# A fused attention and two mixtures of experts: the first two tiles of each mixture taken as early snapshots

## The reference

```python
# attention: 4 batches x 8 heads x 576 positions x 64, block-causal mask (blocks of 64)
attn = softmax(mask(q @ k.T / 8)) @ v
x = attn.transpose(0, 2, 1, 3).reshape(2304, 512)      # N tokens x D

# first mixture: 8 experts, F = 1024, capacity 576
logits = x @ w_gate;  e = argmax(logits);  g = softmax(logits)[e]
# tokens in order: the first 576 of each expert are kept, the others give 0
y = g * (relu(x @ w1[e]) @ w2[e])

# second mixture, on y as x
do = (x @ w_skip) > 0                                  # tokens that are computed at all
out = x;  out[do] = x + g * (relu(x @ w1b[e]) @ w2b[e])
```

## Time and profile before

| | us |
|---|---|
| median of three runs | 697.13 (696.61 to 699.2) |
| the profiled execution | 697.51 |
| its span, first to last instruction | 696.0 |
| PE busy | 675.1 (97%) |
| DVE / ACT / POOL busy | 365.4 / 263.2 / 144.0 |
| a tile of mixture 1, of mixture 2 (steady) | 14.6, 13.1 |
| mean granted TensorE clock | 0.996 |

### The profile page before, as it was taken

How to read it: one execution, slowest core, us unless ns; L and a number is a source line. 1 busy time by engine, 2 the same in 40 slices (tenths; PEclk the granted TensorE clock), 3 DMA queues, 4 the chain that set the end, 5 groups by cost and what they waited for, 6 DMA issues and landing times.

```text
span 696.0 us, 16986 instructions
## 1 busy us (share of the span) xinstructions
PE 675.1 (97%) x5624; PEld 593.1 (85%) x5625; DVE 365.4 (52%) x1019; ACT 263.2 (38%) x642; POOL 144.0 (21%) x236
## 2 busy tenths in 40 slices
PE   7999999999999799999999999999899999999997
PEld 6788888888887699999899988998798989999986
DVE  3767787787877533357633367435612444411144
ACT  5566566566663122244322143123211433411133
POOL 5100021021011313222222222231212112112112
PEclk9999999999999999999999999999999999999999
DMA  8757568658331354110711158871481688701101
GB/s 179 197 144 197 173 164 240 178 148 252 69 101 70 105 201 147 31 46 24 259 42 39 45 193 321 292 282 43 129 301 60 200 312 326 279 30 45 45 17 33
DMA packets 94332, 103.75 MB, mean 149 GB/s; under 512 B 63629, under 2 KB 63629, under 8 KB 94288
## 3 DMA queue, kind: packets, MB, share of 16 engines
q1 hardware_dynamic: 83600, 79.19, 36.5%
q0 software_dynamic: 9072, 22.89, 9.9%
q10 hardware_dynamic: 1616, 1.08, 0.5%
HBM read 83.44 MB, written 26.53 MB: 158 GB/s over the span
## 4 chain that ended last, share of the span: by engine, by line
PE 88%; DMA 5%; DVE 3%; issue 2%; SPq 1%; ACT 0%; POOL 0%; POOLq 0%; ACTq 0%; DVEq 0%
PE ps L1408 29%; PE ps L1415 24%; PE ps L1304 8%; PE ps L1255 6%; PE ps L1279 5%; PE ps L1311 3%; PE ps L1235 3%; DMA rows<-queue 3%; PE ps L1247 2%; PE ps L1386 2%; PE ps L1397 2%; PE ps L1391 1%; PE ps L1272 1%; DMA queue<-pad 1%; DMA kn<-in_k 1%
## 5 line engine op out<-in xcount | busy, mean ns | idle before, releaser
L1408 PEld LDWEIGHTS ps<-xT,w 128*128 128x128 f32 x1344 | 153.8, 192 | 6.8 <-issue 3.5
L1408 PE MATMUL ps<-xT,w 128*128 128x128 f32 x1344 | 155.2, 275 | 3.9 <-issue 1.4
L984 DVE SCALAR_TENSOR_TENSOR hT_lo<-ps,hT_hi 128x512 fp32r<-128x512 f32 x64 | 44.1, 691 | 134.3 <-ACT hT_hi L1160 129.5
L1415 PE MATMUL ps<-w_hi,hT_hi 128*128 128x512 f32 x256 | 105.2, 411 | 1.2 <-DVE hT_lo L984 1.0
L1415 PE MATMUL ps<-w_lo,hT_hi 128*128 128x512 f32 x256 | 100.6, 393 | 0.0
L1415 PE MATMUL ps<-w_hi,hT_lo 128*128 128x512 f32 x256 | 100.2, 391 | 0.0
L1160 ACT ACTIVATE hT_hi<-ps 128x512 fp32r<-128x512 f32 x64 | 37.9, 593 | 133.3 <-PE ps L1408 133.3
L1408 PE MATMUL ps<-xT,w_last 128*128 128x128 f32 x704 | 81.8, 275 | 0.0
L1408 PEld LDWEIGHTS ps<-xT,w_last 128*128 128x128 f32 x704 | 81.0, 192 | 0.9
L1101 ACT ACTIVATE probs<-ps,negmax 128x128 f32<-128x128 f32 (+3 forms) x128 | 65.8, 527 | 22.1 <-DVE negmax L737 22.1
L737 DVE TENSOR_REDUCE negmax<-ps 128x2 f32<-128x256 f32 (+1 forms) x64 | 51.1, 821 | 33.6 <-PE ps L1260 33.6
(11 more groups left out here) (174 smaller groups left out, 886.1 us busy)
## 6 DMA issues: line engine op xcount, KB each, us to landing
w2all<-in_moe_w SPq DMA_DIRECT2D x10, 2048.0 KB, 14.6
w<-in_moe_w SPq DMA_DIRECT2D x7, 2048.0 KB, 9.0
rows<-queue POOLq DMA_DIRECT2D x38, 257.0 KB, 3.0
w2all<-in_moe_w SPq DMA_DIRECT2D x16, 512.0 KB, 5.2
w<-in_moe_w SPq DMA_DIRECT2D x12, 512.0 KB, 3.8
w_last<-in_moe_w SPq DMA_DIRECT2D x3, 2048.0 KB, 9.0
qn<-in_q SPq DMA_DIRECT2D x32, 144.0 KB, 3.7
out<-pad SPq DMA_DIRECT2D x4, 1152.0 KB, 8.8
```

The lines of the kernel that those rows point to most:

```text
L984: vec.scalar_tensor_tensor(out=hT_lo[:, hs, :].bitcast(f32r), in0=hTp[half], scalar=0.0, in1=hT_hi[:, hs, :], op0=ALU.max, op1=ALU.subtrac ...
L1408: last = mm(hTp[half][:, j, :], w1s[slot][:, c, f:f + P], xT[:, c, :], start=(c == 0), stop=(c == DC - 1))
L1415: last = mm(yp, h_[:, j, :].bitcast(f32r), w_[:, j, :].bitcast(f32r), start=(j + n == 0), stop=(j == FC - 1 and n == 2))
```

## The change

What it does:
- The first tiles of **two** experts (0 and 1) of each mixture are tiles 0 and 1 whatever they hold. They are loaded as snapshots before the last routing has placed its rows, and both 128-row stretches are then blanked with pads in the queue. Where the stretch was full at the snapshot, the expert goes on behind it; where it was not, it is visited again from its first row, in which only the later rows are left.
- `find_early` is gone; `find_full` (five small DVE instructions, once a mixture) gives the table which of the two was full.
- PE: tile 0's hidden matmuls stand around the last `rows_back` and ranks, in place of filler; tile 1 is written out ahead of the loop, on every engine; in mixture 1 the transposes of y and the logits stand between eighths of the second hidden half, and the ranks behind the first eighth of the values.
- DVE: the index part of the last routing stands between `split_h` 0 and 1 of tile 0 (mixture 1); `make_table` stands behind both in both mixtures. A tile's routing is cut in two, around `split_h` 1.
- ACT: the last routing's exp stands behind `copy_x`; pads of experts 5 to 7 behind tile 0's two `relu`, in a loop. SP: pads of experts 0 to 4, in a loop.
- POOL: mixture 1's last batch is scattered once both stretches are blanked; `placed` counts the scatters into queue 2 apart from those into `out`.

The core of the diff:

```diff
-            def load_first(phase, found, placed, rows):
+            def load_firsts(phase, there):
+
 
                 p = ph[phase]
-                sp.wait_ge(p.early_ready, found)
-                sp.sem_inc(carried, 1)
-                late = sp.value_load(tab(phase, T_PAD, LATE), min_val=0, max_val=1)
-                sp.wait_ge((scattered, ph[0].scattered)[phase], late * rows + placed)
-                sp.sem_inc(carried, 1)
-                sp.wait_ge(p.first_padded, late * 16 + 16)
-                sp.dma_start(firsts[phase], queues[phase][0:P, :]).then_inc(p.tile0_loaded, 16)
+                sp.wait_ge((scattered, placed)[phase], there)
+                for e in range(FIRSTS):
+                    sp.dma_start(firsts[phase][e], queues[phase][e * REGION:e * REGION + P, :]).then_inc(p.first_loaded[e], 16)
+                for e in range(FIRSTS):
+                    sp.wait_ge(p.first_loaded[e], 16)
+                    sp.dma_start(queues[phase][e * REGION:e * REGION + P, :], pad[:, :]).then_inc(p.blanked, 16)
...
                 p = ph[phase]
                 if phase == 1:
-                    total = sp.value_load(tab(0, T_CUM, E), min_val=1, max_val=NT)
-                    load_first(1, total, total * 32 + (ENDPADS - 32), 16)
-                pad_ends(sp, phase, range(E // 2, E), p.padded)
+                    total = sp.value_load(tab(0, T_CUM, E), min_val=FIRSTS, max_val=NT)
+                    load_firsts(1, total * 16)
+
+                sp.wait_ge(p.blanked, 16 * FIRSTS)
+                pad_ends(sp, phase, 0, E - ACT_PADS, p.padded)
                 sp.wait_ge(p.table_ready, 1)
...
+                pool.wait_ge(p.first_loaded[0], 16)
+                take_row(0, firsts[phase][0][:, kept].unsqueeze(1))
+                if phase == 0:
+
+                    pool.wait_ge(p.blanked, 16 * FIRSTS)
+                    scatter_batch(B - 1)
                 pool.wait_ge(p.rows_ready, 1)
-                first_rows = [row_of(t) for t in range(1, RING + 1)]
+                first_rows = [row_of(t) for t in range(FIRSTS, FIRSTS + RING)]
                 if phase:
-
-                    pool.wait_ge(ph[0].scattered, total * 32 + (ENDPADS - 16))
+                    pool.wait_ge(placed, total * 16 + 16)
                     carry()
                 else:
                     pool.wait_ge(scattered, B * (NI * 16))
                 pool.wait_ge(p.scattered, ENDPADS)
-                pool.wait_ge(p.padded, 16 * (E - 1))
-                pool.wait_ge(p.first_padded, 32)
-                load_rows(first_rows[0], slice(1, 2))
-                if phase:
-                    scatter(out, y2[:, 0:D], idxo[:, 0:1], N - 1, ph[0].scattered)
+                pool.wait_ge(p.padded, 16 * E)
+                load_rows(first_rows[0], slice(2, 3))
+                if phase == 0:
+                    pool.wait_ge(out_cleared, 16 * B)
+                pool.wait_ge(p.first_loaded[1], 16)
+                take_row(1, firsts[phase][1][:, kept].unsqueeze(1))
+                total = pool.value_load(tab(phase, T_CUM, E), min_val=FIRSTS, max_val=NT)
+                for t in range(3, FIRSTS + RING):
+                    pool.wait_ge(p.loaded, 16 * (t - FIRSTS))
+                    load_rows(first_rows[t - FIRSTS], slice(t % RING, t % RING + 1))
+                if phase == 0:
+                    scatter_values(1)
                 else:
-                    pool.wait_ge(out_cleared, 16 * B)
-                pool.wait_ge(p.tile0_loaded, 16)
...
-                signal(ph[phase].early_ready, value)(vec.tensor_scalar(tab(phase, T_PAD, LATE), count, float(P) - 0.5, None, ALU.is_lt))
+            def find_full(count):
+
+                link(vec.tensor_tensor(full[:, 0:FIRSTS], count[:, 0:FIRSTS], base[:, 0:FIRSTS], ALU.subtract))
+                link(vec.tensor_scalar(full[:, 0:FIRSTS], full[:, 0:FIRSTS], float(P) - 0.5, None, ALU.is_ge))
+                link(vec.tensor_tensor(onward[:, :], full[:, 1:E + 1], full[:, 0:E], ALU.subtract))
+                link(vec.tensor_scalar(onward[:, :], onward[:, :], float(P), float(REGION), ALU.mult, ALU.add))
+                link(vec.tensor_scalar(begun[:, :], full[:, 0:1], float(P), None, ALU.mult))
...
-                link(vec.tensor_scalar(n_[:, 0:1], n_[:, 0:1], 1.0, None, ALU.max))
-                vec.tensor_scalar(tabs[phase][:, T_N, 0:1], n_[:, 0:1], -1.0, None, ALU.add)
+                link(vec.tensor_tensor(n_[:, 0:E], n_[:, 0:E], full[:, 0:E], ALU.subtract))
+                vec.tensor_copy(tabs[phase][:, T_N, 0:E], n_[:, 0:E])
 
                 link(vec.tensor_copy(tmp[:, E + 1:2 * E + 1], n_[:, 0:E]))
...
-                vec.tensor_copy(tabs[phase][:, T_CUM, 1:E + 1], cum_[:, 1:E + 1])
-                link(vec.tensor_scalar(tmp[:, 0:E], n_[:, 0:E], -float(P), float(REGION), ALU.mult, ALU.add))
+                vec.tensor_scalar(tabs[phase][:, T_CUM, 1:E + 1], cum_[:, 1:E + 1], float(FIRSTS), None, ALU.add)
+                link(vec.scalar_tensor_tensor(out=tmp[:, 0:E], in0=n_[:, 0:E], scalar=-float(P), in1=onward[:, :],
+                                              op0=ALU.mult, op1=ALU.add))
                 link(vec.tensor_tensor(past[:, :, :], tile_no[:, 0, :].unsqueeze(2).to_broadcast([P, 32, E]),
...
+                        route_end(t)
+
+                        dve.wait_ge(p.y_taken, t)
+                    else:
+
+                        dve.wait_ge(p.scattered, t * 16 + ENDPADS)
+                    finish_tile(t)
+                    dve.sem_inc(carried, 1)
+                    split_next(t, *ahead)
+
+
+                if phase == 0:
+                    split_h(0, 1)
+                    dve.wait_ge(ranks_ready, B)
+                    last_router.take_rows()
+                    last_router.keep_capacity()
+                    dve.wait_ge(x_scaled, 2 * PAIRS)
+                    index_batch(B - 1)
+                    last_router.count_rows()
+                    make_ends(0)
+                    split_h(1, 2)
+                else:
+                    split_h(0, 1)
+                    split_w2(slice(0, 1), 0, range(2, 4))
+                    split_h(1, 2)
+                make_table(phase)
+                total = dve.value_load(tab(phase, T_CUM, E), min_val=FIRSTS, max_val=NT)
                 if phase:
-                    split_w2(0, 0, range(2, 4))
-                split_h(1, 2)
-                total = dve.value_load(tab(phase, T_CUM, E), min_val=1, max_val=NT)
-                if phase:
-                    dve.wait_ge(ph[0].scattered, done * 32 + ENDPADS)
-                else:
-                    find_early(1, count2[0:1, 0:1], 1)
-                ahead = look_ahead(0)
+                    dve.wait_ge(ph[0].scattered, done * 16 + ENDPADS)
+                    dve.wait_ge(placed, done * 16 + 16)
                 finish_tile(0)
-                split_next(0, *ahead)
+                split_w2(slice(1, 2), 4)
+                tile(1)
...
-                    split_w2(0, 0, range(2), ph[1])
-                    route_tile(total, last=True)
+                    find_full(count2)
+
+                    split_w2(slice(0, 1), 0, range(1), ph[1])
+                    route_begin(total)
+                    split_w2(slice(0, 1), 0, range(1, 2), ph[1])
+                    route_end(total)
+                    make_ends(1)
...
+                if phase == 0:
+                    copy_x(1)
+                    act.sem_inc(p.xq_copied, 1)
+                    router_exp(NI, shifted_ready, exps_ready, B)
+                relu(0, 0)
+                relu(0, 1)
+                pad_ends(act, phase, E - ACT_PADS, E, p.padded)
+                copy_x(2)
                 act.sem_inc(p.xq_copied, 1)
-
-                pad_ends(act, phase, range(1, E // 2 - 1), p.padded)
-                relu(0, 0)
-                pad_ends(act, phase, range(E // 2 - 1, E // 2), p.padded)
-                relu(0, 1)
-                copy_next(0, slice(1, 2))
-                copy_x(2)
-                act.wait_ge(p.table_ready, 1)
...
+                        def split_new():
+                            with act.If(first_tile > 0):
+                                split_w2(ds(slot, 1))
+                            with act.Else():
+                                act.sem_inc(p.w2_hi_ready, 4)
+
+                        tile(t, ds((t + 1) % RING, 1), split_new)
...
+                def tile(t, slot):
+                    pe.wait_ge(p.x_copied, t + 1)
+                    hidden(range(0, 4), slot)
+
+                    if phase == 0:
+                        transpose_y(t)
+                        hidden(range(4, 6), slot)
+                        logits_y(t)
+                        hidden(range(6, FC), slot)
+                    else:
+                        pe.wait_ge(p.y_copied, t + 1)
+                        carry()
+                        hidden(range(4, FC), slot)
+                    transpose_x(t + 2)
+                    values_here(t, 0)
+                    values_of(range(0, 1))
```

(86 more changed lines are left out.)

246 lines of the change are left out of this document (89 added, 157 removed).

## The result

The changed kernel takes **713.4 us** (median of 4 runs, 712.55 to 714.07) against 697.8 for the kernel before beside it: ratio **1.0223 [1.0198, 1.0247]**. It is slower, by 15.6 us; 709.5 was forecast, and 713.4 lies in the range.

The account below looks back on a forecast made before the run. PE, busy 97% of the span, was taken to bound the kernel: only its work and waits count. 697.5 - 6.2 + 5.5 + 13.1 = 709.9, less 0.4 to the median, gave 709.5 us; range 700.5 to 715.5.

Parts of the forecast that it names:

- likeliest case: Whole kernel: the forecast of 709.5 us itself, its own range 706.5 to 713, chance 0.60.
- Step 1: Mixture 2: one more tile, for expert 1, which has no row; +13.1 us.
- Rival C: Mixture 2: the added tile is not there, device counts differing from those worked out; 696.4 us, chance 0.05.
- Step 2: Attention to mixture 1: tile 1 starts earlier, less a 2.3 us wait and half clock; gain 6.2 us, bounds 4 and 9.4.
- the clock: Tile 1 of mixture 1: half clock behind PE's wait costs 0.9 us, bounds 0 and 1.7.
- Step 3: Inside mixture 1's tiles: 0, with an upper end of 0.2 us on each of six switches.
- Step 4: Mixture 1 to 2: late row load and scatter make PE wait 8.4 us in tile 2; +5.5 us, bounds -5.0 and +8.5.
- the order on DVE: Mixture 2: make_table behind split_h puts the table's rows at 501.5, where before they were there at 494.8.
- POOL's order: Mixture 2: two more row loads stand ahead of scatter_out(0); 20.8 us from first landing to released PE, less 0.5.
- Rival A: Mixture 2: row loads beside the weights run at their uncontended 3.0 us; total 701.8 us, chance 0.14.
- Rival B: Both mixtures' starts: tile 2's row load, and mixture 2's split, ready before PE wants them; not slower, 695.8 us, chance 0.06.
- Rival D: Pad loops or fresh code delay the row load by 3 more, or half clock costs more in both places; 715, chance 0.15.

Follow-up runs that it names:

- the exchange: The changed kernel with experts 1 and 5 of mixture 2 exchanged (gate columns and weights), so 15 tiles there: ratio 1.0038 to the kernel before.
- the second ratio of the changed kernel: The changed kernel itself, unaltered, measured again as the yardstick for other runs: 712.1 us, ratio 1.0199 to the kernel before.
- the pads unrolled: The changed kernel with the pad loops on SP and ACT written out: 712.51 us, ratio 1.0197 to the kernel before.
- relu-first kernel: The changed kernel with relu and copy_yT ahead of copy_next in every tile on ACT: 720.87 us, ratio 1.0152 to the kernel before.
- table first: The changed kernel with mixture 2's table made ahead of the first split_h: 715.83 us, ratio 1.0247 to the kernel before.
- all but the exchange: The changed kernel with mixture 2's first output scatter and ACT's relu/copy_yT moved ahead, filler back, pads written out, experts not exchanged: 707.04 us, ratio 0.9956 to before.

## Why the prediction was right, and where its terms were off

**The sum.** Forecast +12.4 (709.5 less 697.1), measured +15.6 by the medians and +15.3 by the profiles. The likeliest case had 706.5 to 713 as its own range; the result lies 0.4 above it, inside the range as a whole.

**Step 1, the added tile: right.** 13.1 forecast from the earlier trace rows; 13.0 in the profile's account, 13.0 by the exchange (11.3 with the second ratio of the changed kernel), 12.3 between two kernels on chip C that differ in it and in the pads. Rival C (no added tile) falls. The reading of the input's routing, not of the profile, found it.

**Step 2, attention to mixture 1: mechanism right, the clock mis-sized.** Tile 1 starts at 235.9, even earlier than the 237.3 forecast, 10.5 before 246.5: the sum had all 7.4 us of hidden matmuls behind `rows_back`, though its first eighth (1.1 us) stands ahead of it. The wait for `copy_yT` was 3.1 (forecast 2.3: the row load went out at 239.8 and not 240.6, but PE was there 1.4 earlier). The term that failed is the clock: I took 0.9, bounds 0 and 1.7, from a stretch of 3.4 us at half clock; it lasted 6.6 us and cost 3.3. It is not a fixed price either: behind the same wait of 3.1 it was 3.4 us with the pads unrolled. The gain was 4.3 instead of 6.2. The relu-first kernel shows that wait and clock went together: without the wait, tile 1 is 6.6 us shorter.

**Step 3, inside the tiles: right.** Mixture 1's other tiles add up to the same time; 14.58 each, with mostly up to 0.2 more where a tile begins an expert. One of these takes 15.3, where before had one of 16.2; the equal sums owe something to that.

**Step 4, mixture 1 to 2: +5.5 forecast, +6.7 measured, right in size and in the place of the wait, wrong on which edit held the first row load.** On a clock that starts at the end of mixture 1: hidden begins at 6.4 (forecast 7.1), ends are written at 12.0 (10.9), the table's rows are there at 21.1 (20.3), the row load goes out at 25.0 (22.6) and lands at 27.9 (25.6), PE is at its wait at 39.7 (37.5), is released at 46.4 (45.9), and tile 3 starts at 58.5 (57.5). I wrote that "the edit that costs is the order on DVE". That step fell: table first moved the rows 3 us and the row load not at all. What held it were ACT's three pads, 1.93 us apart where I priced 1.5, behind a second `relu` that the half clock had made late, the last of them 3.7 us from issue to landing where I had 2.7. My own sum had them behind the table by 1.5; they were behind it by 3. That the size came out within 1.2 is partly luck: the row load landed 2.3 later than forecast, but from its landing to the released PE it took 18.6 us and not 20.3, since the second row load took 4.8 where before had 6.9, so the release was only 0.5 late. From there to tile 3 it was 12.0 instead of 11.6: the hidden half at half clock (5.9, forecast 5.3) did not hide under DVE's split, which was over 0.4 us before PE began the values. The wait was 6.7 rather than 8.4, since PE came later too: the half clock behind the snapshot (3.68 for sixteen matmuls) and 0.8 for `split_h` in tile 1.

**POOL's order: right.** This was the costlier part, 9.2 of the 22.3 us of tile 2, and one moved call takes it back.

**Rival A**, row loads at 3.0 beside the weights, falls: they took 4.8 and 6.5 (before 6.9 and 6.4), against 2.9 and 3.4 for the first of each mixture. By the Trainium skill's "DMA: Bandwidth & Descriptors", section "Anatomy of one DMA — SWDGE (gpsimd) path", the estimate was 2.6 for each: 0.3 to 0.8 short of the first loads, and 2.2 and 3.9 short of the two beside the weights; the measurement decides. **Rival B** falls as a result of this kernel, but its mechanism is real. (Its "12.4 us earlier than the forecast has it" is wrong: 12.4 is the distance from 514.5 to the forecast's y at 526.9; the forecast's scatter, 3.9 ahead of y as in rival A, is 8.5 from it.) It was to decide from a scatter issued earlier, and with that, the relu and the filler put right, the kernel with all but the exchange is at 0.9956, near the 695.8/697.1 = 0.998 of rival B. **Rival D**'s half clock "in both places" is most of the difference between 709.5 and 713.4: 2.4 us by the price of the clock in the first place alone. For its loops nothing was seen, since unrolling gave nothing that could be measured; its fresh code was not tested.

What stays open: why a pad on ACT's queue takes 3.7 us to land here and 2.4 at the attention (the 2.7 of the forecast was one on POOL's queue), why SP's three pads of mixture 1 need 5.6 us on chip A and 8.5 on chip B, and what decides how long the clock stays at half behind a given wait.

## What to carry to other kernels

Work that is made unconditional to start it early costs its full length where the data make it empty: count the tiles on the real input first. When a load is taken off the path, look at what still waits for it by its place in an in-order queue: here a copy (ACT) and a scatter (POOL) that needed nothing of the row loads stood behind them, and moving the two calls, with some filler ahead of mixture 2 (and the pads unrolled, which showed no gain), turned +2% into -0.4% with the added tile and -2.2% without. A hole in PE is priced with the clock behind it, which here doubled it and in another kernel added half.

## What the runs showed of the hardware that was not expected

- The stretch at half clock is not one length, and the same wait does not always bring it. Read in steps of 0.2 us around the two changes of stage, the thirteen profiles have 28 stretches at the 1.2 GHz level: twelve of 3.4 us, fifteen of 6.8 and one of 10.2, parts of them while PE still waited. The wait of 3.1 in tile 1 of mixture 1 was followed by a stretch of 6.8 in the changed kernel and of 3.4 with the pads unrolled. The wait of 1.8 to 1.9 ahead of that tile was followed by one of 3.4 in four kernels and by none in two (exchange, and all but the exchange), where I had drawn the line between 1.1 and 2.7.
- What differs in one stage of two single profiles can therefore be the clock: both tiles that looked 1.4 to 1.5 us shorter by the unrolled pads had the same wait and 3.4 us less of half clock.
- An iteration of the pads' loop on ACT with its transfer took 1.93 us, 0.55 of it one register load from the table (495.66 to 497.57 in the chain). From the first issue to the end of the third, three took 4.2 us in the loop and 3.8 written out.
- The attention, whose code was the same, ended at 222 to 224 us on chip A and at 231 to 233 on chips B and C, in every kernel, while the steady tiles of the changed kernel (14.58 and 13.04) agreed to 0.01.
